# Filling work ahead of layer 1: products of zeros in place of turnings of the identity

## What is computed

```python
# q, k, v: 4 batches, 8 heads, 576 positions, 64 wide
scores = scale * q @ k.T, masked to 0 <= pos_q - pos_k < 64
attn = softmax(scores) @ v                    # -> x: 2304 tokens, 512 wide
h = max(max(x @ w1, x @ w2), x @ w3)          # layer 1: 512 -> 768; h @ w_out: 768 -> 512
h = h @ moe2_w_in                             # 512 -> 2048
g = where(h >= 1, h, where(h <= -1, 0, (h + 1)**2 / 4))
out = g @ moe2_w_out                          # 2048 -> 512
```

## Time and profile before

| | |
|---|---|
| runs | 748.91 us median (748.75 to 750.69) |
| the profiled execution | 749.52 us |
| its span, first to last instruction | 747.7 us |
| TensorE busy | 740.5 us, 99% |
| ScalarE, GpSimd, VectorE busy | 330.3, 313.8, 300.4 us |
| first record of TensorE | 1.53 us |
| first matmul of layer 1 | 21.31 us |

### The profile page before, as it was taken

The page is one execution under the profiler, slowest core; times in us unless marked ns, Lnnn a source line. Parts: engine busy times, 40 slices in busy tenths (PEclk is TensorE's granted clock), DMA queues, the critical chain, the costliest instruction groups (busy, mean ns, idle before and its releaser), DMA issues.

```text
span 747.7 us, 12711 instructions
## 1 busy us (share of the span) xinstructions
PE 740.5 (99%) x4731; PEld 657.0 (88%) x4731; DVE 300.4 (40%) x744; ACT 330.3 (44%) x795; POOL 313.8 (42%) x239
## 2 busy tenths in 40 slices
PE   8999999999999999999999999999999999999997
PEld 6998888888888888999998989989899898998986
DVE  3542342143132023354047532644644453266324
ACT  6764543434430111454256552474554455245332
POOL 5741121111110520566067762576774376257321
PEclk9999999999999999999999999999999999999999
DMA  9652331121101200120011020011210004001302
GB/s 340 238 201 76 109 97 59 60 87 30 30 1 53 88 1 1 33 79 0 0 57 58 0 85 1 1 72 42 74 69 2 1 1 150 19 2 57 113 1 85
DMA packets 24040, 46.18 MB, mean 62 GB/s; under 512 B 2224, under 2 KB 3632, under 8 KB 23984
## 3 DMA queue, kind: packets, MB, share of 16 engines
q1 hardware_dynamic: 23552, 44.93, 17.7%
q10 hardware_dynamic: 432, 0.49, 0.2%
HBM read 37.55 MB, written 7.86 MB: 61 GB/s over the span
## 4 chain that ended last, share of the span: by engine, by line
PE 98%; DVE 1%; DMA 0%; ACT 0%; issue 0%; SPq 0%; DVEq 0%
PE wide L540 30%; PE wide L619 26%; PE bank L599 24%; PE wide L572 10%; PE wide L502 3%; PE bank L526 3%; PE bank L511 2%; PE wide L547 1%; DVE part_in L965 0%; DMA q<-q_dram 0%; ACT prob L641 0%; DVE prob L849 0%; ACT pT L656 0%; SPq L416 0%; DVE xT L836 0%
## 5 line engine op out<-in xcount | busy, mean ns | idle before, releaser
L540 PE MATMUL wide<-xT,w 128*128 128x512 f32 (+1 forms) x1080 | 234.7, 373 | 0.0
L540 PEld LDWEIGHTS wide<-xT,w 128*128 128x128 f32 x1080 | 186.3, 188 | 34.7 <-issue 2.1
L619 PE MATMUL wide<-w4s,gT 128*128 128x512 f32 x864 | 205.6, 391 | 0.0
L619 PEld LDWEIGHTS wide<-w4s,gT 128*128 128x128 f32 x864 | 161.3, 188 | 32.1 <-POOL gT L1016 0.4
L1016 POOL TENSOR_TENSOR gT<-g,gT 128x384 fp32r<-128x384 f32 x96 | 111.6, 1173 | 175.1 <-ACT gT L636 175.1
L599 PE MATMUL bank<-yT,w3s 128*128 128x384 f32 x1008 | 183.6, 336 | 0.0
L599 PEld LDWEIGHTS bank<-yT,w3s 128*128 128x128 f32 x1008 | 177.2, 188 | 4.1 <-DVE g L957 0.3
L939 DVE TENSOR_TENSOR pu<-bank,pu 128x384 f32<-128x384 f32 x72 | 40.1, 557 | 174.8 <-PE bank L599 172.9
L1024 POOL TENSOR_TENSOR prob<-prob,row_inv 128x512 f32<-128x512 f32 x36 | 38.2, 1064 | 153.6 <-DVE row_inv L855 153.6
L762 ACT ACTIVATE g_sq<-g_sq,half 128x384 f32<-128x384 f32 x96 | 58.9, 616 | 85.4 <-DVE g_sq L951 83.4
L869 DVE TENSOR_TENSOR h<-wide,h 128x512 f32<-128x512 f32 (+1 forms) x60 | 38.0, 634 | 94.9 <-PE wide L540 94.8
(11 more groups left out here) (54 smaller groups left out, 538.6 us busy)
## 6 DMA issues: line engine op xcount, KB each, us to landing
v<-v_dram SPq DMA_DIRECT2D x36, 256.0 KB, 3.8
raw<-w_dram SPq DMA_DIRECT2D x16, 512.0 KB, 3.5
h<-moe_w_dram SPq DMA_DIRECT2D x12, 384.0 KB, 6.3
k<-k_dram SPq DMA_DIRECT2D x16, 288.0 KB, 4.7
q<-q_dram SPq DMA_DIRECT2D x16, 256.0 KB, 4.3
part_dram<-o_sb SPq DMA_DIRECT2D x12, 256.0 KB, 2.0
part_in<-part_dram SPq DMA_DIRECT2D x2, 1536.0 KB, 6.9
out_dram<-part_in SPq DMA_DIRECT2D x11, 256.0 KB, 2.1
```

Source lines behind the costliest of these rows:

```text
L540: mm = pe.matmul(acc[gr % 2][:, 0:cols], w123[:, wp, w, kc, c * P:(c + 1) * P], xT[:, x_side(t), xp, kc, 0:cols], start=(kc == x == 0), st ...
L619: mm = pe.matmul(acc4[b], gT[:, k, gp, tb * P:(tb + 1) * P], w4s[pair_f(g) % HALF_F][:, wp, f, :], start=(first and x == 0), stop=(last an ...
```

## The change

VectorE's stream begins with a memset of a new 128x128 tile, `blank`, to zero, which counts up the semaphore `blanked`. `turn_identity` becomes `turn_blank`: each of its N is a plain float32 product of `blank` with itself (128x128 by 128x128) into the same PSUM bank, instead of a transpose. TensorE's stream begins behind `blanked` instead of behind the constants; the wait for the constants moves to the first `probs`. Of the counts, the first goes from 12 to 15, those between the scores from 2 to 4 each, and the one ahead of probs0 from 10 to 8; the later ones (8, 8, 2, 7) stay. The outputs are the same.

```diff
--- before.py
+++ after.py
@@ -123,7 +123,7 @@
         v7 k8 q8 v8 v9 v10 v11 w8 w9 w10 w11 k9 q9 v12 v13 k10 q10
     """,
     "PE": """
-        turn12 score0 turn2 score1 turn2 score2 turn10 probs0 score3 values0 probs1 turn8 values1 probs2 turn8
+        turn15 score0 turn4 score1 turn4 score2 turn8 probs0 score3 values0 probs1 turn8 values1 probs2 turn8
         values2 turn2 probs3 turn7 values3 score4 group0 group1 score5 group2 probs4 group3 group4 probs5 group5 values4 score6 group6 probs6 group7
         probs7 group8 values5 score7 group9 probs8 group10 group11
     """,
@@ -257,6 +257,7 @@
     pT, at = place("pT", [P, PROBS, NB * P], F32, at)
     mask, at = place("mask", [P, 3, SPAN], F32, at)
     ident, at = place("ident", [P, P], F32, at)
+    blank, at = place("blank", [P, P], F32, at)
     tiny, at = place("tiny", [P, 8], F32, at)
     neg_max, at = place("neg_max", [P, PROBS, NB], F32, at)
     row_sum, at = place("row_sum", [P, PROBS, NB], F32, at)
@@ -315,7 +316,7 @@
     w_in = [sem(f"w_in{piece}") for piece in range(3 * KC)]
     wo1_in = sem("wo1_in")
     w3_in, w4_in = sem("w3_in"), sem("w4_in")
-    ident_zero, consts = sem("ident_zero"), sem("consts")
+    ident_zero, consts, blanked = sem("ident_zero"), sem("consts"), sem("blanked")
     w_hi = [sem(f"w_hi{piece}") for piece in range(3 * KC)]
     w_lo = [sem(f"w_lo{piece}") for piece in range(3 * KC)]
     scored, maxed, exped = sem("scored"), sem("maxed"), sem("exped")
@@ -505,6 +506,8 @@
             mm.then_inc(scored, 1)
 
         def probs(s):
+            if s == 0:
+                pe.wait_ge(consts, CONSTS)
             pe.wait_ge(normed, s + 1)
             after(pe, p_copied, s)
             for i in range(NB):
@@ -542,14 +545,14 @@
                                    start=(kc == x == 0), stop=(kc == KC - 1 and x == 2))
             mm.then_inc(l1_done, 1)
 
-        def turn_identity(count):
+        def turn_blank(count):
             for _ in range(count):
-                pe.transpose(acc[1][:, 0:P], ident[:, :], ident[:, :])
-
-        pe.wait_ge(consts, CONSTS)
+                pe.matmul(acc[1][:, 0:P], blank[:, :], blank[:, :], start=True, stop=True)
+
+        pe.wait_ge(blanked, 1)
         for kind, i in in_order("PE"):
             if kind == "turn":
-                turn_identity(i)
+                turn_blank(i)
             elif kind == "score":
                 score(i)
             elif kind == "probs":
@@ -831,6 +834,8 @@
 
     @block.vector
     def _(dve):
+        dve.memset(blank[:, :], 0.0).then_inc(blanked, 1)
+
         def lo(dst, src, high):
 
             return dve.tensor_tensor(dst, src, high.bitcast(F32), ALU.subtract)
```

## The result

| | before | changed |
|---|---|---|
| median | 749.23 us (748.29 to 750.69, 6 runs) | 753.42 us (752.8 to 754.1, 6 runs) |
| ratio to before | | 1.0053 (1.0042 to 1.0064) |
| profiled execution, its span | 749.52, 747.7 us | 753.44, 751.3 us |
| first record of TensorE | 1.53 us | 1.05 us |
| score0 | 4.60 us | 6.50 us |

The account below looks back on a forecast made before the run. TensorE's stream, without waits from 15.36 us on, was taken to bound the kernel. Adding 0.6 us up to values1 and 1.8 us behind it, +2.4 us, to the profiled 749.52 gave 751.9 us, range 750.2 to 754.0.

Parts of the forecast that it names:

- What bounds the kernel: Whole run: TensorE never waits from 15.36 us on, so each added nanosecond in its stream moves the end by one.
- What a filling product costs: Each filling product: two records, 0.218 us at full clock and 0.43 at half, against 0.109 and 0.217 for a turning.
- The upper bound of 0.26 us a product: Costlier filling products, two rounds at the cold score's 0.265 us: would bring the total to 753.3 us.
- (a): Start of TensorE: it waits for VectorE's memset instead of the identity, beginning at 1.0 us, a gain of 0.5 us.
- (b): First filling: 30 records, clock rising at 4.5 us (4.2 to 6.7), score0 at 6.1 us instead of 4.60.
- (c): Around the scores: 1.5 us from score to score against 1.67; probs0 starts 0.6 us later than its 10.75.
- (d): From probs0 to values1: all slides by 0.6 us, values1 to 16.0; idle 1.09 us hides the longer turn8.
- (e): From values1 to layer 1: 17 more records without cover, 1.85 us, of which 1.8 us are left.
- a rise as late as 10.3 us: Rival at the head: the clock does not rise earlier, probs0 3.6 us late, total 754.9 us; chance 0.10.
- The sum was not too large: Rival: clock rises at 2 to 3 us, or waiting hides more filling; 749.5 to 751.2, say 750.5 us; chance 0.16.
- The cheap product: Rival on the fillings: a product costs no more than a turning, layer 1 1.6 us earlier, 747.9 us; chance 0.05.
- Double-length records: Rival on the fillings: each record takes two turnings, 0.436 us a product, above 757 us; chance 0.03.

Follow-up runs that it names:

- turn_id: Changed kernel with its counts, but each filling again a one-record turning of the identity and TensorE starting behind the constants; 748.98 us, ratio 0.9999.
- late_half: Changed kernel with the four late fillings cut from 8, 8, 2, 7 to 4, 4, 1, 3 products; 751.59 us, ratio 1.0044.
- turns30: Kernel before with 30 turnings of the identity ahead of score0 instead of 12; 750.18 us, ratio 1.0024.
- before_again: Kernel before, unchanged, run for a second trace; 748.51 us.
- before_third: Kernel before, unchanged, run for a third trace; 748.06 us.
- mixed: Changed kernel with 8 products of zeros as first filling, then turnings in the counts of the kernel before; 748.47 us, ratio 1.0002.
- fit: Changed kernel with products of zeros fitted to the waits, 8, 1, 1, 7, 4, 4, 1, 3; 748.68 us, ratio 0.9998.
- none: Kernel before with all filling counts set to 0; 752.04 us, ratio 1.0045.

## Why the prediction was right, and where it was not

It gave 751.9 us, 750.2 to 754.0, slower at 0.75; measured were 753.42 us, 4.2 above the kernel before. The direction and the term that decides it came from the right working. Of the size, 2.4 us were forecast and 3.9 measured between the two profiled executions.

*What bounds the kernel*: held. TensorE still has no wait behind 16.97 us, and the span moved with the start of layer 1 to 0.1 us in every run of the table.

*What a filling product costs*: held, and it decides. Two records a product, 0.213 us apart at the low level and 0.111 at full clock, where 0.109 was taken. turn_id takes the second record away, and with it the loss. The upper bound of 0.26 us a product would have given 753.3 us, nearly the measured time, but a product takes 0.22; that agreement would have been luck.

*(a)*: the memset took 0.17 us from 0.83 on, TensorE began at 1.05; forecast 1.0.

*(b)*: score0 at 6.50, forecast 6.1. The clock rose at 5.1 instead of the 4.5 taken, half of which is 0.3 us; the rest is the start at 1.05, the spacing of 0.111 and a longer first spacing.

*(c)*: this term was mis-sized. From score to score it is 8.19 - 6.50 = 1.69 us, forecast 1.5: score0 to the next start took 0.60 us instead of 0.53, the filling 1.09 instead of 0.97. The 0.53 was half of a slow score's time, which holds for the records but not for the change of form between scores and filling. Together with (b), probs0 came 1.61 us later than in the earlier trace rows instead of 0.6.

*(d)*: held. values1 slid by the same 1.61 us as probs0, and the longer turn8 ahead of it went into the idle 1.09, of which 0.17 is left.

*(e)*: held. 24.86 - 16.97 less 21.31 - 15.36 is 1.94 us, forecast 1.8; late_half got 1.87 of it back.

Sum: 1.61 + 1.94 = 3.55 instead of 2.4 us. Of the 1.15 us that the sum missed, 1.0 lie in (b), (c) and the filling ahead of probs0, and 0.14 in (e); what is left of the measured 3.9 lies outside the span.

*The reason given for the clock was wrong.* Step (b) said "if products count for it and turnings don't", and worked the moment of the rise out from the three scores alone. turns30 and before_again show that turnings count, so the rise at 5.1 us is no earlier than the kernel before has it in two of three traces (4.5, 5): that the estimate of 4.2 to 6.7 us held is luck of the arithmetic. The rule of the Trainium skill that was set beside it (TensorE: Matmul & The Clock Gate, Part 4: PE-mode transpose, that transpose mode doesn't count as busy in the same way) disagrees with these traces: the spacing halved, from 0.217 to 0.112 us, within a row of 30 turnings. The factor of four that the Trainium skill gives for the transpose mode (TensorE: Matmul & The Clock Gate, Terms) disagrees too: turnings and the records of products stand 0.109 and 0.111 us apart, and with two records the factor is two.

*The yardstick was a late execution*, with 10.3 us against 4.5 and 5 in the two others. Against before_third the change costs at score0 1.90, at probs0 2.99, at values1 2.93 and at layer 1 4.87 us: all that the clock seemed to give back in the sum came from the yardstick. The forecast of the time itself did not suffer by it, since it was added up from starts in the changed kernel; what suffered is the account of what the change costs. What holds for the medians lies between the two, since the kernel before has late executions among its runs. The prediction noted that this execution lay 0.6 us above the median and drew nothing from it.

The rivals: a rise as late as 10.3 us was seen in neither trace of the changed kernel, and its seven executions took 754.1 us at most, where such a rise was priced at 754.9. The sum was not too large either: the rise came at 5.1 us and not at 2 to 3, and late_half shows no wait that the late fillings cover. The cheap product fell with the count of records. Double-length records fell with their spacing.

## What to carry to other kernels

Count records, not calls: a plain float32 product is two records on TensorE where a transpose of the same size is one, and filling in a stream that bounds the kernel costs its full length once the waits that it stands in are used up. Size each filling in microseconds against the wait that it covers, at the pace that the clock has there: without any of it layer 1 began 3.6 us later than in before_third, with too much 4.9 us later. And where a profile shows a stretch that hangs on the moment at which the clock rises, take two or three traces of the unchanged kernel before a sum is built on one.

## What was not expected of the hardware

- The granted clock rose between 4.2 and 6.2 us in all but one of the traces with filling, whether this consisted of turnings or products, of zeros or the identity, and at 10.3 us in that one, although its work up to 4.6 us was the same, record for record, as in before_third. What makes an execution late stays open. Going by the spans, it shows in a third of the executions of the kernel before, in one of mixed, and in none of the 7 of the changed kernel or the 11 of fit.
- The column of the granted clock gave 1.00 for the head although records stood 0.213 us apart there instead of 0.11; only the spacing tells.
- Where the filling is missing, TensorE ran at the low level with pauses of 0.6 to 1.3 us between its short pieces until it had been in layer 1 for about 2 us (none): the first 24 matmuls took 1.0 us more than at full pace, which is 2 us at half pace.
